# 48 semaphore increments behind the last scatter in Pool's program

## The reference

```
e_idx = np.argmax(x @ w_gate, axis=1)
for e in range(E):
    mask = e_idx == e
    h = np.maximum(x[mask] @ w1[e], 0.0)
    out[mask] = gate_w[mask, None] * eom[mask, e, None] * (h @ w2[e])
```

## Time and profile before

| what | value |
|---|---|
| median of three runs | 1031.67 us |
| the profiled execution, whole | 1031.78 us |
| its span, first to last instruction | 1030.2 us |
| granted TensorE clock, mean | 0.997 |
| TensorE busy | 98% of the span |
| Pool busy | 24% of the span |

### The profile page before, as it was taken

How to read it: one execution, slowest core, us unless ns; L and a number is a source line. 1 busy time by engine, 2 the same in 40 slices (tenths; PEclk the granted TensorE clock), 3 DMA queues, 4 the chain that set the end, 5 groups by cost and what they waited for, 6 DMA issues and landing times.

```text
span 1030.2 us, 24331 instructions
## 1 busy us (share of the span) xinstructions
PE 1012.4 (98%) x7343; PEld 839.0 (81%) x7344; DVE 548.7 (53%) x1141; ACT 395.1 (38%) x731; POOL 248.1 (24%) x457
## 2 busy tenths in 40 slices
PE   7999999999999999999999999999999999999997
PEld 5788888888888888888878888888888888888885
DVE  6786766667676767666546534233342432442521
ACT  6544434444344344344332433233343322432421
POOL 5861302112021212021323222222222222222211
PEclk9999999999999999999999999999999999999998
DMA  9442222222112222210014444233232331341110
GB/s 325 153 163 83 79 77 83 83 83 79 43 60 77 83 83 73 83 63 31 22 52 150 156 143 151 94 114 122 72 127 87 122 123 41 104 137 43 39 36 31
DMA packets 41601, 97.17 MB, mean 94 GB/s; under 512 B 8254, under 2 KB 8382, under 8 KB 41536
## 3 DMA queue, kind: packets, MB, share of 16 engines
q1 hardware_dynamic: 32000, 75.28, 22.0%
q0 software_dynamic: 9248, 20.70, 6.4%
q10 hardware_dynamic: 288, 0.27, 0.1%
HBM read 76.66 MB, written 20.60 MB: 94 GB/s over the span
## 4 chain that ended last, share of the span: by engine, by line
PE 94%; issue 2%; DMA 1%; DVE 1%; ACT 1%; POOL 0%; SPq 0%; POOLq 0%; DVEq 0%; ACTq 0%
PE Y_ps L478 39%; PE H_ps L478 39%; PE X L470 8%; PE S L470 3%; PE X L625 2%; PE S L609 2%; PE L_ps L596 1%; PE L_ps L478 1%; DMA stage<-in_experts 0%; DMA stage<-in_q 0%; DMA xg<-x_rows,slot_rec 0%; POOL route_table L1445 0%; DVE dl L1011 0%; DMA route_table<-rec,posi 0%; SPq L427 0%
## 5 line engine op out<-in xcount | busy, mean ns | idle before, releaser
L478 PE MATMUL Y_ps<-wx,dh 128*128 128x512 f32 (+1 forms) x1184 | 377.0, 399 | 1.0 <-DVE dl L1011 1.0
L478 PE MATMUL H_ps<-wx,xh 128*128 (+1 forms) x960 | 263.0, 396 | 0.5 <-DVE xl L1011 0.2
L478 PEld LDWEIGHTS Y_ps<-wx,dh 128*128 128x128 f32 x1184 | 213.6, 188 | 43.3 <-DVE dl L1011 1.9
L478 PE MATMUL Y_ps<-wx,dl 128*128 128x512 f32 (+1 forms) x592 | 231.7, 391 | 0.0
L478 PEld LDWEIGHTS H_ps<-wx,xh 128*128 128x128 f32 x960 | 175.6, 188 | 35.0 <-issue 1.3
L478 PE MATMUL H_ps<-wx,xl 128*128 (+1 forms) x480 | 148.0, 389 | 0.0
L1011 DVE TENSOR_TENSOR dl<-X,dh 128x512 fp32r<-128x512 f32 x152 | 97.7, 683 | 90.3 <-ACT dh L784 90.0
L1011 DVE TENSOR_TENSOR wx<-stage,wx (+1 forms) x58 | 70.3, 1224 | 119.4 <-ACT wx L977 119.3
L478 PEld LDWEIGHTS Y_ps<-wx,dl 128*128 128x128 f32 x592 | 111.1, 188 | 24.5
L478 PEld LDWEIGHTS H_ps<-wx,xl 128*128 128x128 f32 x480 | 90.1, 188 | 19.2
L784 ACT ACTIVATE dh<-X 128x512 fp32r<-128x512 f32 x152 | 81.8, 592 | 7.5 <-DVE i_load L1330 4.4
(11 more groups left out here) (213 smaller groups left out, 1136.3 us busy)
## 6 DMA issues: line engine op xcount, KB each, us to landing
stage<-in_experts SPq DMA_DIRECT2D x64, 512.0 KB, 3.5
stage<-in_q SPq DMA_DIRECT2D x36, 256.0 KB, 3.8
stage<-in_v SPq DMA_DIRECT2D x36, 256.0 KB, 3.6
x_rows<-x SPq DMA_DIRECT2D x36, 256.0 KB
stage<-in_k SPq DMA_DIRECT2D x35, 256.0 KB, 4.7
stage<-in_moe_w_out SPq DMA_DIRECT2D x4, 512.0 KB, 6.5
stage<-in_moe_w_in SPq DMA_DIRECT2D x3, 512.0 KB, 6.2
slot_rec<-route_table POOLq DMA_DIRECT2D x40, 2.0 KB, 2.3
```

The lines of the kernel that those rows point to most:

```text
L478: i = pe.matmul(acc[:, c0:c0 + HALF], x[:, kk, :], w(part, kk * cols + c0), start=first and x is hi and part == 0, stop=last and x is lo)
```

## The change

Behind the written-out last steps of Pool's program, and so behind the last scatter, 48 increments of `passed` are added. Nothing else is touched.

```
--- before.py
+++ after.py
@@ -1513,6 +1513,8 @@
                 slot(c + 1, 0, lambda k: True)
             for u in range(1, 5):
                 slot(last, u, lambda k: u + k < 4)
+            for _ in range(48):
+                pool.sem_inc(passed, 1)
 
 
```

## The result

The changed kernel takes 1033.83 us, the median of 18 runs, beside 1031.68 us for the kernel before in the same runs. The ratio is 1.0016 with a 95% interval of 1.001 to 1.0023, so it is 1.0 to 2.4 us slower: by the ratio 1.7 us, by the two medians 2.15. The interval leaves 1 out, so there is a difference. But it is no more than about the 0.2%, 2.06 us, under which the prediction calls a time unchanged. The forecast was 1031.9, +0.27 us.

A forecast was written before the change was run, and what follows sets the result against it. Pool's closing DRAIN was taken to end the span: 48 increments at 0.08 us start it at 1030.16, plus 0.05 ends it at 1030.21 instead of 1029.94, +0.27 us, so 1031.9 us; range 1031.3 to 1034.5.

The forecast's parts named there:

- Rival (a): Pool's closing DRAIN works rather than waits: 2.41 us of its own behind the increments, +2.6 us, 1034.3; chance 0.12.
- Rival (b): The longer Pool program needs one more code fetch, stalling the sequencer among the increments: +2.7 us, 1034.4; chance 0.08.
- two signs: Forecast wrong if the time leaves 1031.5 to 1032.9 us; its mechanism wrong if Pool's closing DRAIN stays long.
- What ends the span: At the program's end Pool arrives last, 0.5 us behind SyncE; the end of its DRAIN, 1029.94, sets the time.
- The price of one increment: On Pool's sequencer, distance from one increment to the next: 0.08 us, so 48 take 3.84 us.
- The overlap: Pool's sequencer runs the increments from 1026.32 while the last scatter proceeds; without overlap the cost would be +1.5 us.
- What is left of the DRAIN: Pool's closing DRAIN, starting at 1030.16 behind the increments with nothing left to wait for, takes 0.05 us.
- The break-even of 74 ns: Price per increment at which the 48 behind the last scatter would begin to delay the end of Pool's DRAIN.
- The threshold given for it, 2.1 us: The DRAIN's own time above which its working, not waiting, was said to decide the outcome.
- Rival (c): The stall ahead of the last scatter hangs on the program's end and vanishes: -2.2 us, 1029.5; chance 0.14 in full.
- Rival (d): The increments reach Pool's sequencer merged or left out: 0 change, 1031.7; counted inside the forecast's 0.64.
- V2: Follow-up theory: a Pool DRAIN takes about 1.2 us plus 0.057 us per DMA since the start, whatever was drained before.

## Why the prediction was right, and where it was off

The time of 1033.83 us lies within the stated range, 1031.3 to 1034.5, and the change is small, as forecast, because the increments do run beside the scatter. But the range is that wide because it takes in rivals (a) and (b). By the two signs that the prediction set for itself it fails: the time left 1031.5 to 1032.9, the range of its own mechanism, and the DRAIN stayed long, 1.21 us instead of under 0.1. That the loss still passes for no change is in part luck: 1.36 us of tail, or 2.15 between the medians, stand beside a limit of 2.06.

- **What ends the span** held. SyncE's DRAIN starts at 1030.2 in the changed kernel and Pool's ends at 1032.0; in the runs with 16 to 96 increments behind the scatter only Pool's last pieces move.
- **The price of one increment** held: 0.08 forecast, 0.078 measured, 3.76 us in all instead of 3.84. The page's row of a wait followed by a register move was a good stand-in for a run of bare increments.
- **The overlap** held. The increments start at 1027.07, before the scatter's record at 1027.29, and the scatter lands 2.8 us behind its start as in the earlier trace rows. So the Trainium skill's rule (PSUM — Partial Sum Buffer, "Engine vs sequencer instructions"), that the sequencer waits only for dispatch, agrees with this trace.
- **What is left of the DRAIN** was the term that was mis-sized: "So 0.05 us". It measured 1.21 us in the changed kernel, and this is nearly the whole error: 3.54 + 1.21 = 4.75 us behind the scatter's start, where the forecast made it 1030.21 - 1026.55 = 3.66, and 3.39 before. The three DRAINs that the step rested on the earlier trace rows were of other engines, or of Pool before its first DMA. None stood behind DMAs that Pool had issued, and the forecast saw that only as rival (a). The break-even of 74 ns was an error of the same term: with 1.21 us it lies at 31 increments of 0.078, not at 46.
- **Rival (a)** had the right place, a DRAIN that takes time of its own, and twice the size: it read all 2.41 us behind the record as work. The threshold given for it, 2.1 us, was wrong by the prediction's own sum: with d for the DRAIN's own time, the end moves by 1030.16 + d - 1029.94, which passes 2.06 us at d = 1.84. The 1.21 measured lie below either.
- **Rival (b)** didn't come with 48 increments: they stand evenly 0.078 us apart, no halt among them. It had a real thing in view, though. With 96, 0.34 us are lost once, behind the 87th, beside the stand of 2.45 us that the rival priced. The rule that code comes in blocks and that crossing a boundary costs, though mostly hidden (the Trainium skill, Runtime: NRT & Kernel Launch, "Instruction fetch mechanics"), agrees with that if the halt is such a crossing; the transfer beside it is one of 8 KB, not of the page's 16 KiB.
- **Rival (c)** fell in its premise. The stall doesn't hang on the program's end, since it stands unchanged in front of the increments. It hangs on what Pool has issued by DMA before, which the one more DMA showed; whether it counts DMAs, rows or something else isn't shown. The reason given for its being systematic ("the four times lie within 0.35 us") was weak: 18 runs of the same kernel spread over 4.6 us. The stall itself was the same to 0.01 us in every trace that had it.
- **Rival (d)** fell: the trace has all 48 records.

## What to carry to other kernels

Instructions behind the last work of an engine are free only as far as what follows them has nothing of its own to do, and a wait that looks idle can hide such a part. No other DRAIN gave the price of the closing one here: those of other engines, or ahead of the first DMA, were too short, and those in mid-program far too long. Different counts of increments ahead of it did: with 16 the end didn't move, with 36 the DRAIN was down to its own 1.21 us. A stall marked "issue" that is the same in every trace is a lead worth more than the change at hand: here one more small DMA, or a DRAIN placed in idle time shortly before the end, took 2.4 to 2.9 us off the tail where the change added 1.4. To find what such a stall hangs on, move one thing at a time under it: code ahead, time between, then the count of DMAs. And hold a rule drawn from added instructions against those that were there all along: the closing DRAIN of the kernel before already spoke against V2.

## What the runs showed of the hardware that was not expected

- Pool's sequencer takes 2.95 us instead of 0.52 to issue its 165th DMA of the program, shown for the last scatter and, with one more DMA ahead, for the one before it; at the 123rd the record is 1.70 us long instead of 1.02. A DRAIN of Pool one or two DMAs ahead removes the halt at the 165th; one behind the 37th DMA removes the halt at the 123rd and leaves that at the 165th.
- A DRAIN put into Pool's program behind DMAs is not cheap: 3.33 us at 483 us, 10.45 and 10.51 us near the end, 47 ns when repeated at once. The closing one, behind all 165 DMAs, takes 3.62 us.
- 96 increments in a row show one halt of 0.34 us, behind the 87th, 0.7 us ahead of a transfer of instructions; 48 show none.
- The last DRAIN has 1.21 us of its own, or 0.21 us when another started 22 us before it, and so the same 48 increments cost 1.36 us of tail in one case and 0.87 in the other (3.75 - 2.88).
